# Mixture of experts in groups of up to 416 rows with stationary weights and transposed results, instead of slots of 128 rows

## The reference

```
cur   = u * k_t (outer) v_t
y_t   = r_t . (state + cur)
state = w * state + k_t (outer) v_t
```

```
logits = x @ w_gate                       # (3072, 8)
e      = argmax(logits, axis=1)
gate   = softmax(logits)[e]
out[n] = gate[n] * (relu(x[n] @ w1[e]) @ w2[e])     # 384 -> 1024 -> 384
```

```
h = x @ w_in;  g = max(0.01 * h, h);  return g @ w_out
```

## Time and profile before

| | |
|---|---|
| median of 3 runs | 947.4 us (947.17 to 949.24) |
| span of the profiled execution, first to last instruction | 946.8 us |
| time of the profiled execution outside its span | not shown |
| PE busy | 879.3 us, 93% of the span |
| VectorE busy | 384.6 us |
| ScalarE busy | 255.5 us |
| GpSimd busy | 354.8 us |
| DMA moved | 81.26 MB, mean 86 GB/s |

### The profile page before, as it was taken

How to read it: one execution, slowest core, us unless ns; L and a number is a source line. 1 busy time by engine, 2 the same in 40 slices (tenths; PEclk the granted TensorE clock), 3 DMA queues, 4 the chain that set the end, 5 groups by cost and what they waited for, 6 DMA issues and landing times. The chain is left out here.

```text
span 946.8 us, 16037 instructions
## 1 busy us (share of the span) xinstructions
PE 879.3 (93%) x5167; PEld 800.8 (85%) x5168; DVE 384.6 (41%) x793; ACT 255.5 (27%) x469; POOL 354.8 (37%) x355
## 2 busy tenths in 40 slices
PE   4999999963999999999994899999999999999997
PEld 3899999962889898989893688889889889889887
DVE  5757787661322223232322432523423423324332
ACT  1223323310222222222221232332332333232322
POOL 7675557553567765393774910010010010000000
PEclk9989999985999999999997799999999999999999
DMA  7657656415434453342433300010010010000000
GB/s 153 149 126 193 166 136 162 112 60 175 152 95 152 148 162 97 119 151 80 160 122 109 108 26 18 34 29 6 33 33 0 33 33 0 33 0 1 33 1 34
DMA packets 113789, 81.26 MB, mean 86 GB/s; under 512 B 80608, under 2 KB 107616, under 8 KB 113760
## 3 DMA queue, kind: packets, MB, share of 16 engines
q1 hardware_dynamic: 101760, 59.21, 22.5%
q10 hardware_dynamic: 8928, 12.21, 4.2%
q0 software_dynamic: 3072, 9.45, 3.0%
HBM read 56.46 MB, written 24.40 MB: 85 GB/s over the span
## 5 line engine op out<-in xcount | busy, mean ns | idle before, releaser
L1338 DVE TENSOR_TENSOR gl<-gf,gh 128x512 fp32r<-128x512 f32 x96 | 66.7, 694 | 258.1 <-ACT gh L1300 258.1
L150 POOL TENSOR_TENSOR w_lo<-stage,w_hi 128x768 fp32r<-128x768 f32 (+1 forms) x70 | 145.7, 2081 | 5.8
L1296 ACT ACTIVATE hc<-bank 128x512 f32<-128x512 f32 x96 | 57.4, 598 | 271.8 <-PE bank L1244 271.8
L1262 PE MATMUL bank<-w_hi,gh 128*128 128x384 f32 x384 | 130.7, 340 | 0.0
L1262 PE MATMUL bank<-w_lo,gh 128*128 128x384 f32 x384 | 129.8, 338 | 0.0
L1262 PE MATMUL bank<-w_hi,gl 128*128 128x384 f32 x384 | 129.8, 338 | 0.0
L1244 PE MATMUL bank<-xh,w_hi 128*128 128x512 f32 x288 | 116.3, 404 | 4.4 <-DVE xl L1325 4.4
L1244 PE MATMUL bank<-xl,w_hi 128*128 128x512 f32 x288 | 115.2, 400 | 0.0
L1244 PE MATMUL bank<-xh,w_lo 128*128 128x512 f32 x288 | 114.8, 399 | 0.0
L1208 POOL DMA_INDIRECT xg<-z_rows,pos_i x24 | 23.0, 958 | 237.4 <-PE bank L1231 213.5
L984 PE MATMUL bank<-w_hi,ht_hi 128*128 x224 | 78.0, 348 | 1.3 <-DVE ht_lo L1110 1.3
(11 more groups left out here) (151 smaller groups left out, 1461.4 us busy)
## 6 DMA issues: line engine op xcount, KB each, us to landing
stage<-in_moe_w SPq DMA_DIRECT2D x24, 512.0 KB, 3.2
stage<-in_moe_w SPq DMA_DIRECT2D x32, 384.0 KB, 3.4
z_rows<-pad_row SPq DMA_DIRECT2D x20, 384.0 KB, 3.2
xs<-x_rows ACTq DMA_DIRECT2D x30, 192.5 KB, 2.4
z_rows<-ys ACTq DMA_DIRECT2D x28, 192.0 KB, 1.9
rn<-in_r SPq DMA_DIRECT2D x48, 96.0 KB, 2.4
kn<-in_k SPq DMA_DIRECT2D x48, 96.0 KB, 2.7
vp<-in_v SPq DMA_DIRECT2D x48, 96.0 KB, 2.6
```

What stands on the lines that cost most here:

```text
L150: i = eng.tensor_tensor(w_lo[:, buf, off:off + cols], stage[:, h, 0:cols], w_hi[:, buf, off:off + cols].bitcast(F32), ALU.subtract)
L1262: i = pe.matmul(ps_o[t][:, 0:D], x[:, f % NB, t * P:(t + 1) * P], ww[:, 1, o:o + D], start=f == 0 and x is gh and ww is w_hi, stop=f == FF ...
L1296: act.activation(hc[:, f % 2, :], ps_h[f % 2][:, :], ACT.Copy).then_inc(h_ok, 1)
L1338: dve.tensor_tensor(gl[:, f % NB, :], gf[:, f % 2, :], gh[:, f % NB, :].bitcast(F32), ALU.subtract).then_inc(gl_ok, 1)
```

## The change

The attention block writes no zeros to `z_rows`, multiplies each row by its gate before the row is written (`gates`, on ScalarE), and puts the token's number where the gate was (`tok_no`, plus 256 per use of a buffer). The tables are those of groups instead of slots; an expert with more than 416 rows gets more than one group, and an odd number of groups is made even. A region has 416 spare rows, and the zeros behind the last row of each expert are now written in the next block.

The expert and dense blocks become one. A group has up to 416 rows, loaded as four tiles of 104 partitions. Now the weights are stationary and the transposed rows move, 416 columns at a time: in step f, `hidden` gives 128 hidden columns in transposed form, which after relu and split are at once the moving operand of `output`, two steps behind; the hidden rows are not transposed back. The results stay transposed in SBUF (`z_t`, by running row number), from where VectorE splits them for the dense stage; the gather and its transposes go. The last two steps of a group's `output` follow the next group's `transposes`. ScalarE moves the column of token numbers, group by group, into one list in DRAM (`move_ids`), and the list is loaded once. GpSimd then scatters the final rows by token number (`scatter`), in place of one store per group. `x_split` stands in the middle of a dense group instead of its end. The step of the dense stage is otherwise as before. Core of the diff:

```diff
+    U = 416
+    TR = U // 4
+    MORE = (N - 1) // U
+    LOOKS = E + MORE + 3
+    RR = N + U
+    assert U % 8 == 0 and TR <= P
...
-                    at = c * (2 * HP) + 2 * q
-                    dst = z_slots[at:at + 2] if isinstance(c, int) else z_slots[bass.ds(at, 2)]
-                    sp.dma_start(dst.rearrange("s p d -> p s d"),
-                                 pad_row[:, 0:D].unsqueeze(1).broadcast_to([P, 2, D])).then_inc(filled, 16)
-                sp.wait_ge(consts, 9)
+                sp.wait_ge(consts, 11)
+                sp.dma_start(x_rows[0:U, :].rearrange("(t p) d -> p t d", p=TR),
+                             pad_row[0:TR, :].unsqueeze(1).broadcast_to([TR, U // TR, XW])).then_inc(filled, 16)
...
-                    pool.wait_ge(route, c * RS + (2 * RS - 1))
+                    pool.wait_ge(route, c * RS + 2 * RS)
                     if not isinstance(c, int):
                         carry_wait(pool, 1)
+                    pool.wait_ge(gated, c * B + B)
+                    if not isinstance(c, int):
+                        carry_wait(pool, 3)
...
+                def gates(c, par):
+                    act.wait_ge(route, c * RS + 8)
+                    for b in range(B):
+                        act.activation(yc[:, par, b, 0:D], yc[:, par, b, 0:D], ACT.Copy,
+                                       scale=gate[:, par, b:b + 1]).then_inc(gated, 1)
...
+                        pool.wait_ge(l2_mm, n * FC - FC)
+                        carry_wait(pool, 2)
+                    for i, piece in enumerate(expert_pieces(0)):
+                        split_piece(pool, n * NPE + i, (b * NPE + i) % 2, b, piece, i in ENDS)
...
+                def scatter(g):
+                    for t in range(G):
+                        if t < 2:
+                            pool.wait_ge(o_act, g * 2 + t + 1)
+                        else:
+                            pool.wait_ge(o_dve, g * 2 + t - 1)
+                        idx = ids_i[:, g * G + t:g * G + t + 1]
+                        pool.indirect_dma_start(out, bass.IndirectOffsetOnAxis(ap=idx.bitcast(U32), axis=0),
+                                                rows[:, t, 0:D], None).then_inc(stored, 16)
...
+                pool.wait_ge(l2_mm, last * FC)
+                carry_wait(pool, 2)
+                for n, piece in enumerate(w_in_pieces()):
+                    split_piece(pool, base + n, n % 2, 0, piece, n == NPI - 1)
+                base = base + NPI
+                pool.wait_ge(h_mm, pairs * (2 * FC))
+                carry_wait(pool, 2)
+                for n, piece in enumerate(w_out_pieces()):
+                    if n == NPO // 2:
+                        pool.wait_ge(l2_mm, pairs * (2 * FC))
+                        carry_wait(pool, 2)
+                    split_piece(pool, base + n, n % 2, 1, piece, False)
...
+                def transposes(n):
                     pe.wait_ge(x_loaded, n * 16 + 16)
                     for d in range(DC):
...
+                        for t in range(4):
+                            i = pe.transpose(ps_x[d][:, t * TR:(t + 1) * TR], rows[0:TR, t, d * P:(d + 1) * P],
+                                             ident[0:TR, 0:TR])
+                        i.then_inc(xt_mm, 1)
...
+                def hidden(n, b, f):
+                    if not isinstance(n, int) or n > 0 or f >= 2:
+                        pe.wait_ge(h_lo_ok, n * FC + (f - 1))
+                    if f == 0:
+                        pe.wait_ge(parts_ready, n * 2 + 1)
+                    for d in range(DC):
+                        if f == 0:
+                            pe.wait_ge(xt_lo_ok, n * DC + (d + 1))
+                        o = d * FE + f * P
+                        for ww, x in ((w_hi, x_hi), (w_lo, x_hi), (w_hi, x_lo)):
+                            i = pe.matmul(ps_h[f % 2][:, 0:U], ww[:, b, o:o + P], x[:, b, d, 0:U],
+                                          start=d == 0 and ww is w_hi and x is x_hi, stop=d == DC - 1 and x is x_lo)
+                    i.then_inc(h_mm, 1)
...
+                def output(n, b, f):
+                    if f == 0:
+                        pe.wait_ge(parts_ready, n * 2 + 2)
+                        if not isinstance(n, int) or n > 0:
+                            pe.wait_ge(y_copied, n * DC)
+                    pe.wait_ge(h_lo_ok, n * FC + (f + 1))
+                    for d in range(DC):
+                        o = DC * FE + f * D + d * P
+                        for ww, h in ((w_hi, h_hi), (w_lo, h_hi), (w_hi, h_lo)):
+                            i = pe.matmul(ps_y[d][:, 0:U], ww[:, b, o:o + P], h[:, f % NB, 0:U],
+                                          start=f == 0 and ww is w_hi and h is h_hi, stop=f == FC - 1 and h is h_lo)
+                        if f == FC - 1 and d < DC - 1:
+                            i.then_inc(y_mm, 1)
+                    i.then_inc(l2_mm, 1)
...
+                def group(n, b):
+                    transposes(n)
+                    if not isinstance(n, int) or n > 0:
+                        for f in range(FC - LAG, FC):
+                            output(n - 1, 1 - b, f)
                     for f in range(FC):
...
+                        hidden(n, b, f)
+                        if f >= LAG:
+                            output(n, b, f - LAG)
+                pairs, last = pairs_of(pe), last_of(pe)
+                group(0, 0)
+                group(1, 1)
+                with pe.Fori(1, pairs) as t:
+                    group(t * 2, 0)
+                    group(t * 2 + 1, 1)
+                for f in range(FC - LAG, FC):
+                    output(last, 1, f)
...
+                def move_ids(n):
+                    row, off = entry(act, group_row, n, E * RR - U), entry(act, group_off, n, N)
+                    if not isinstance(n, int) or n > 0:
+                        act.wait_ge(ids_moved, n * 16)
+                    act.dma_start(id_rows[bass.ds(off, U), :], x_rows[bass.ds(row, U), D:D + 1],
+                                  allow_slow_non_contiguous=True).then_inc(ids_moved, 16)
+                def pad(e):
+                    end = entry(act, end_i, e, e * RR + N)
+                    dst = x_rows[bass.ds(end, U), :].rearrange("(t p) d -> p t d", p=TR)
+                    act.dma_start(dst, pad_row[0:TR, :].unsqueeze(1).broadcast_to([TR, U // TR, XW])).then_inc(padded, 16)
+                def group(n, b):
+                    first = isinstance(n, int) and n == 0
                     for d in range(DC):
...
+                        act.wait_ge(xt_mm, n * DC + (d + 1))
+                        act.activation(x_hi[:, b, d, 0:U], ps_x[d][:, 0:U], ACT.Copy).then_inc(xt_hi_ok, 1)
+                    if not first:
+                        load_x(n + 1)
+                        move_ids(n)
+                    for f in range(FC):
+                        act.wait_ge(h_mm, n * FC + (f + 1))
+                        act.activation(h_hi[:, f % NB, 0:U], ps_h[f % 2][:, 0:U], ACT.Relu).then_inc(h_hi_ok, 1)
+                        if first and f < E // 2:
+                            pad(2 * f)
+                            pad(2 * f + 1)
+                    if first:
+                        act.wait_ge(padded, 16 * E)
+                        load_x(1)
+                        move_ids(0)
...
+                def store_y(n):
+                    off = entry(dve, group_off, n, N)
                     for d in range(DC):
...
+                        if d < DC - 1:
+                            dve.wait_ge(y_mm, n * (DC - 1) + (d + 1))
+                        else:
+                            dve.wait_ge(l2_mm, n * FC + FC)
+                        dve.tensor_scalar(z_t[:, d, bass.ds(off, U)], ps_y[d][:, 0:U], 1.0, None,
+                                          ALU.mult).then_inc(y_copied, 1)
+                def group(n, b):
+                    for d in range(DC):
+                        dve.wait_ge(xt_hi_ok, n * DC + (d + 1))
+                        dve.tensor_tensor(x_lo[:, b, d, 0:U], ps_x[d][:, 0:U], x_hi[:, b, d, 0:U].bitcast(F32),
+                                          ALU.subtract).then_inc(xt_lo_ok, 1)
+                    if not isinstance(n, int) or n > 0:
+                        store_y(n - 1)
+                    for f in range(FC):
+                        dve.wait_ge(h_hi_ok, n * FC + (f + 1))
+                        dve.scalar_tensor_tensor(h_lo[:, f % NB, 0:U], ps_h[f % 2][:, 0:U], 0.0,
+                                                 h_hi[:, f % NB, 0:U].bitcast(F32), ALU.max,
+                                                 ALU.subtract).then_inc(h_lo_ok, 1)
...
+                def x_split(g, b):
+                    for d in range(DC):
+                        z = z_t[:, d, g * (G * P):(g + 1) * (G * P)] if isinstance(g, int) else \
+                            z_t[:, d, bass.ds(g * (G * P), G * P)]
+                        dve.tensor_scalar(x_hi[:, b, d, :], z, 1.0, None, ALU.mult).then_inc(xh_ok, 1)
```

(30 more changed lines are left out.)

622 lines of the change are left out of this document (193 added, 429 removed).

## The result

The changed kernel takes 894.9 us in the median of 4 runs (893.75 to 896.82) where the kernel before takes 947.3 beside it; the ratio is 0.9446 (0.9431 to 0.9462). The forecast was 889.0 with a range of 870 to 908. The profiled execution took 895.5 us, its span 893.8; 1.7 us lie outside the span, where the forecast had taken 0.6.

A forecast was written before the change was run, and what follows sets the result against it. The tensor engine (PE) sets the time. 228.4 + 218.9 + 8.4 + 1.6 + 2.5, + 9.7 stop, + 7 seam, + 403.2 + 1.5 dense, + 7.2 tail = 888.4 us span; plus 0.6, 889.0 us, range 870 to 908.

The forecast's parts named there:

- the stop at group 1's rows: In group 0, PE waits 6.2 us for group 1's load of rows; with 3.5 us of half clock, 9.7 us.
- Expert groups: Expert stage: eight groups, 1152 matmuls at 0.190 us, 218.9 us; transposes 8.4 us; residue for waits and register loads 1.6 us.
- Seam of attention and experts: Between the stages: block ends 2.8 us earlier, 1.8 us given back; first hidden matmul at 228.4.
- Pads and the second load: Group 0: group 1's load waits for eight pads, 5.13 MB at 295 GB/s; rows at 261.0, needed at 254.8.
- pushback: Rival: pads block ScalarE's queue, evictions late in group 0, stop about 24 us in all: 903 us; chance 0.17.
- Nothing else is late inside a group: Inside expert groups, evictions, result copies and splitting stay hidden: 21.2 us of GpSimd splitting against 28.8 us of PE.
- supply: Rival: splitting is slowed so that an expert group lasts 32 us, 7 x 3.2 more: 911 us; chance 0.05.
- Seam of experts and dense: Between the stages: VectorE's split beside GpSimd's and queued copies cost 5 us, plus 2 for a clock drop: 7 us.
- the two short waits that I had named as signs: At the dense stage's start, PE waits 1.5 and 2.4 us on VectorE's split of inputs 1 and 2.
- Dense stage: Six dense groups of 67.2 us, 403.2 us, plus 1.5 us for splitting the next tile.
- End: After PE's end, GpSimd scatters four tiles, the last landing 3.8 us after issue; tail grows from 4.9 to 7.2 us.
- Attention: Attention stage: dropped fills and ScalarE's added gate products change the time by zero.

The follow-up runs named there:

- experiment 8: The changed kernel run again with nothing edited: 888.1 us, ratio 0.9389 to the kernel before.
- Experiment 5: Changed kernel with only pad 1 ahead of group 1's load, the other pads one at a time in later steps and group 1: 879.1 us, ratio 0.9264.
- experiment 2: Changed kernel without the moves of row numbers and their reading back, an iota in their place: 884.8 us, ratio 0.9350.
- experiment 3: Changed kernel with row numbers written to DRAM from the loaded rows in SBUF instead of DRAM to DRAM: 894.1 us, ratio 0.9452.
- experiment 4: Changed kernel with row numbers turned by four transposes into one row and written as one 1.7 KB piece: 890.7 us, ratio 0.9411.
- experiment 9: Changed kernel with gate products made for only 4 of a row's 384 numbers: 884.5 us, ratio 0.9354.
- experiment 10: Kernel of experiment 6 with VectorE's add to the row numbers moved behind the sum of the first pair of heads: 871.6 us, ratio 0.9223.
- experiment 6: Changed kernel with the edits of experiment 4 and Experiment 5 together: 873.4 us, ratio 0.9220.
- experiment 7: Changed kernel with the attention stage's gate products moved behind the sixth copy-out of their chunk: 884.5 us, ratio 0.9326.
- experiment 11: Kernel of experiment 10 with the gate products also moved behind the sixth copy-out: 871.9 us, ratio 0.9222.
- experiment 12: Kernel of experiment 10 with GpSimd splitting w_out only after VectorE has split the first dense tile: 871.1 us, ratio 0.9195.

## Why the prediction was right, and where it was not

The time and the mechanism came out, the stop at group 1's rows above all; but the sum is this close by luck too, since an expert stage 7.3 us late and a dense stage 4.3 us early set each other off in part, and the same kernel took 888.1 us in experiment 8. Term by term, in the trace of the first job (us; the sum of the differences is 5.4, the span 893.8 for 888.4):

| step | forecast | measured |
|---|---|---|
| first hidden matmul | 228.4 | 229.3 |
| PE reaches group 1's transposes | 254.8 | 258.3 |
| their rows landed | 261.0 | 269.1 |
| stop | 6.2 | 10.8 |
| half clock behind it | 3.5 | 2.6 |
| experts end | 469.5 | 476.8 |
| seam to the dense stage | 7 | 8.3 |
| six dense groups | 404.7 | 400.4 |
| tail after PE | 7.2 | 8.3 |

*Expert groups: right.* 1152 matmuls, eight groups, a pitch of 0.188 against 0.190 (2.3 us less in all), transposes of 1.23 us. The 275.6 us of the expert stage before became 247.5 (229.3 to 476.8), and by pitches, transposes and residue alone it would be 216.6 + 8.6 + 1.6 = 226.8. Of the 53.0 us by which the span is shorter, the expert stage thus gives 28.1. From its end to PE's last matmul (505.0 to 942.0 before, 476.8 to 885.5 now) another 28.3 are gained, by the seam and the transposes that went; the tail takes 3.5 back.

*Seam of attention and experts: right in sum.* The load was issued at 221.1, 2.9 us earlier than before; its rows came 5.9 us later, near 227.0, and the gain was given back but for 0.1 us.

*Pads and the second load: the right mechanism, too small.* I had ended the pads at 255.7 by a rate of 295 GB/s for them; the load was issued at 262.9, and in 233.5 to 262 the engines moved 256 GB/s. The load then took 6.2 us, not 3.5: the term "3.5 for the load" was read off a 512 KB piece and the queue was not empty of weights: from 262 to 269 us the engines moved 212 GB/s, more than twice what this load alone makes. The rival "pushback" was part of it: pairs of pads held ScalarE 2.07 to 2.98 us (1.1 to 1.2 of it the two issues, the rest mostly the read of the second row number), and two late evictions cost PE 2.46 us. Experiment 5 shows that both go with the pads' place: with one pad ahead, neither is there.

*Nothing else is late inside a group: wrong.* I held 21.2 us of splitting against 28.8 of PE and priced the moves of row numbers at nothing, without a row for them. They land in 10 us and double the landing of the pieces beside them, GpSimd waits 5 to 6 us a group for the pieces (35.5 us from 285 to 476 us), and the 7 us of slack were used up: 2.33 us of waiting in this job, none in the next. Experiments 2 to 4 settle it: not the row load, not the source, but the 416 separate small writes. The rival "supply" was near it but had another cause: splitting was not slowed, it took (146.6 + 64.8) / 70 = 3.02 us a piece as before; it began late. And it cost a few us, not 22, since the slack covered nearly all.

*Seam of experts and dense: right in size by luck, by another cause.* The split by VectorE beside GpSimd was slow just as forecast (1.82, 1.57, 2.57, 1.56, 2.56 us in this trace), but hidden: the last piece of w_in was 5.8 us late, and the two short waits that I had named as signs are not there. Where the supply is in time (experiments 2, 5, 9, 10), PE waits 2.4 to 3.3 us on x_lo, against the forecast's 3.9; in 4, 6, 7 and 11, where GpSimd's pieces met fewer of VectorE's instructions, 0.2 to 0.6; and experiment 12 takes it away. The granted clock was 0.56 in the 4 us behind the wait, some 1.7 us.

Of the Trainium skill's rule on this ("SBUF — State Buffer", Who interferes with whom: such a pair of instructions excludes each other for a whole one), experiment 12 is the direct test, and it agrees: 2.22 and 1.34 us beside GpSimd, 0.69 alone.

*Dense stage: 4.3 us too much.* Groups of 66.73 us, and the 1.5 us for splitting the next tile cost nothing. The pitch of 512 columns is 0.229 us here, 0.233 before; why is open.

*End: 1.1 us too little.* The last scatter is issued 3.2 us behind PE's end (888.75), as forecast, but the span ends 5.0 us behind it, not 3.8. (The forecast's own times give 7.0 us for this tail, not 7.2.)

*Attention, put at zero: nearly.* A chunk is 1.2 us longer in this trace: (172.20 - 110.58) / 2 = 30.8, before 29.6; in experiment 8's trace it is 0.7. The add to the row numbers, 0.96 us beside GpSimd, seems to be some 0.5 of it (experiment 10), ScalarE's products none (9 and 11); the rest is open. It was paid back: PE's stop at 40 us was shorter and the clock in 44 to 48 was 0.75, not 0.50, so the stage ended 0.6 us later than before.

## What to carry over

Count a DMA by its pieces and by what shares the engines with it, not by its bytes: 1.7 KB in 416 writes slowed the weights more than 640 KB of rows did. When one queue also evicts, a DMA issue, the read of its address or a wait for a landing is a wait for everything behind it: put single issues between evictions, and only what the next load needs ahead of it. When the work of the bounding engine is cut, look at the slack of its supplier again: it decides how much of the gain stays, and in the two traces of the changed kernel its waits on PE differed by 3.3 of the 6.8 us between them.

## What the runs showed of the hardware

- 416 writes of 4 bytes landed in 10.1 us in the median of eight moves (8.5 to 11.0), and 512 KB pieces beside them in 7.1 us where they take 3.3 without the moves (experiment 2); the same numbers in one piece of 1.7 KB left them at 3.2 (experiment 4).
- The issue of a 640 KB pad took ScalarE 0.55 to 0.60 us throughout. Reading a row number from SBUF into a register of ScalarE took 0.28 us ahead of the first pad and 1.22 to 1.92 us from the third on, while the DMA engines were busy (share 0.85 from 240 to 260 us); no run shows whether the load of the engines or the issue just ahead is the cause.
- Where VectorE and GpSimd both worked on SBUF in experiment 10, VectorE's instructions ended 0.28 us (copies) or 0.53 to 0.56 us (subtractions) behind the end of GpSimd's.
- A stretch of half clock near 44 to 52 us comes or stays away from one trace to the next: the granted clock is 0.50 to 0.52 there in the kernel before and in experiments 2, 5, 7 and 9, 1.00 in 4, 6 and 8. The first scatter is at 83.3 to 83.9 us with it and at 79.5 to 81.0 without or with a short one: some 3.5 us. The changed kernel has 0.75 and 1.00 in one trace and 1.00 in the other, so it does not hang on the edits; what decides it is open.
- 416 columns take 0.188 us from start to start, between 0.176 at 384 and 0.229 to 0.233 at 512.
